# Attention in rounds of waves: Z filled in place in two sets of tiles, scaled keys in halves, new orders of steps

## The reference, cut to what matters

```python
def _attn_ref(q, k, v, beta):            # 4 batches x 8 heads, 768 steps, head size 48
    k_n = k / (np.linalg.norm(k, axis=-1, keepdims=True) + 1e-06)
    state = 0
    for t in range(S):
        y[t] = q[t] @ state
        state = state + beta[t] * outer(k_n[t], v[t] - k_n[t] @ state)

x = attention                            # 3072 tokens x 384
h = x @ w_in;  x = (h * tanh(softplus(h))) @ w_out          # dense stage, 2048 wide
P = exp(x @ w_gate), scaled 8 times by rows and columns
out = sum over 8 experts e of P[:, e] * (relu(x @ w1[e]) @ w2[e])
```

## Time and profile before

| | |
|---|---|
| median of 3 runs (lowest to highest) | 2361.82 us (2361.77 to 2361.85) |
| the profiled execution: time, span | 2361.32 us, 2359.5 us |
| mean granted clock of TensorE | 0.998 |
| busy: TensorE, its weight loads | 2341.0 us (99%), 1960.6 us (83%) |
| busy: VectorE, ScalarE, GpSimd | 1281.0, 838.2, 385.9 us |
| attention, up to its last own matmul | about 0 to 386 us |

### The profile page before, as it was taken

One profiled execution on the slowest core, in us unless ns is written; L12 is line 12 of the kernel. 1 busy time (PEld: TensorE's weight loads), 2 busy tenths in 40 slices (PEclk: granted clock), 3 DMA queues, 4 the chain that ended last, 5 costly groups with the idle time before them and its releaser, 6 DMA issues.

```text
span 2359.5 us, 38749 instructions
## 1 busy us (share of the span) xinstructions
PE 2341.0 (99%) x15924; PEld 1960.6 (83%) x15924; DVE 1281.0 (54%) x2496; ACT 838.2 (36%) x1865; POOL 385.9 (16%) x318
## 2 busy tenths in 40 slices
...
GB/s 95 52 58 61 50 48 56 41 0 0 0 0 28 35 1 56 41 14 45 10 54 41 14 48 7 54 41 14 50 5 54 41 14 50 9 50 43 16 35 68
DMA packets 101298, 82.29 MB, mean 35 GB/s; under 512 B 75136, under 2 KB 82048, under 8 KB 99200
## 3 DMA queue, kind: packets, MB, share of 16 engines
...
q10 hardware_dynamic: 144, 0.20, 0.0%
...
## 4 chain that ended last, share of the span: by engine, by line
PE 93%; DVE 5%; issue 1%; ACT 0%; DMA 0%; POOL 0%; SPq 0%; DVEq 0%; ACTq 0%
PE ex_h L160 46%; PE ex_y L160 45%; PE ex_logits L160 2%; DVE at_X L569 1%; DVE at_gram L512 1%; DVE de_w_lo L908 1%; DVE de_en L923 1%; DVE de_hg L936 1%; PE ex_y L629 0%; DVE de_g_lo L916 0%; DVE at_gram L514 0%; DVE de_en L921 0%; DMA at_k_in<-k 0%; DVE at_Z L572 0%; DVE at_gram L559 0%
## 5 line engine op out<-in xcount | busy, mean ns | idle before, releaser
L1372 DVE SCALAR_TENSOR_TENSOR ex_r_lo<-ex_h,ex_r_hi 128x512 fp32r<-128x512 f32 x384 | 264.3, 688 | 928.5 <-ACT ex_r_hi L1249 928.1
L1249 ACT ACTIVATE ex_r_hi<-ex_h 128x512 fp32r<-128x512 f32 x384 | 229.8, 599 | 1283.8 <-PE ex_h L160 1283.8
L160 PE MATMUL ex_h<-x_hi,ex_w_lo 128*128 128x512 f32 x1152 | 448.7, 389 | 0.0
L160 PE MATMUL ex_h<-x_hi,ex_w_hi 128*128 128x512 f32 x1152 | 448.7, 389 | 0.0
L160 PE MATMUL ex_h<-x_lo,ex_w_hi 128*128 128x512 f32 x1152 | 448.5, 389 | 0.0
L160 PE MATMUL ex_y<-ex_r_lo,ex_w_hi 128*128 128x512 f32 x1152 | 448.2, 389 | 0.0
L160 PE MATMUL ex_y<-ex_r_hi,ex_w_lo 128*128 128x512 f32 x1152 | 448.2, 389 | 0.0
L160 PE MATMUL ex_y<-ex_r_hi,ex_w_hi 128*128 128x512 f32 x1152 | 448.1, 389 | 0.0
L1199 POOL TENSOR_TENSOR ex_w_lo<-ex_stage,ex_w_hi 128x512 fp32r<-128x512 f32 x90 | 115.7, 1287 | 1674.6 <-ACT ex_w_hi L1231 1636.5
L160 PEld LDWEIGHTS ex_h<-x_hi,ex_w_hi 128*128 128x128 f32 x1152 | 216.3, 188 | 45.1 <-issue 0.2
L160 PEld LDWEIGHTS ex_h<-x_hi,ex_w_lo 128*128 128x128 f32 x1152 | 216.3, 188 | 44.9
...
## 6 DMA issues: line engine op xcount, KB each, us to landing
...
```

The source lines that it names most:

```text
L160: return nc.tensor.matmul(out, lhsT, rhs, start=start, stop=stop)
L1249: nc.scalar.activation(r[0][:, j, :], h_bank[j][:], ACT.Relu).then_inc(hi_ready, 1)
L1372: nc.vector.scalar_tensor_tensor(out=r[1][:, j, :], in0=h_bank[j][:], scalar=0.0, in1=r[0][:, j, :].bitcast(F32), op0=ALU.max, op1=ALU.sub ...
```

## The change

Z2 and Z become one array of tiles, a set for even and one for odd waves: ZZ writes the 2x2 blocks into Z, and all products read Z. Step Z0 becomes like the other merges: only the second half of each pair of columns is computed and copied. ZZ now waits for the correction of the wave two before (which frees the set) instead of the Z0 of the wave before. GpSimd scales the keys in two halves, each with a semaphore of its own and a wait for two of the four B4 products; F1.u waits for half u only. The addition of 1e-6 goes from VectorE to ScalarE, behind the root. In the first wave VectorE squares 10 heads and GpSimd 6 instead of 8 and 8; ZZ.2 of the first wave goes from VectorE to GpSimd. Two warm-up matmuls less. `beta_t` lies at another address. The lists of all engines in head, round and last are new. In the round, among others: GpSimd has a rest step (RT.3) between the halves of the keys; the grams of groups 2 and 3 are taken at the beginning of VectorE's next round; on SP loadv comes ahead of loadk. In the last part h1 stands ahead of the last residues (res) instead of behind the last W, and xhi of wave 11 behind g.1 on ScalarE. The numbers of steps of each kind are as before, but for single eZ and eres that change between VectorE and ScalarE (VectorE has 45 eZ instead of 39, of which 5 are Z0, and 20 eres instead of 21).

```diff
 ATTENTION_ROUND = {
     "PE": (
-        "res.1@-1 X5.3@-1 Z5.2@-1 res.0@-1 T5.3@-1 corr.1@-1 res.2@-1 Z5.3@-1 corr.0@-1 F2.3:13 corr.2@-1 H.1 "
-        "res.3@-1 H.0 B2.1@-1:0 H.2 X0.1 X0.0 B2.0@-1:1 T0.0 corr.3@-1 T0.1 B1.1:0 X0.2 Z0.0 Z0.1 B2.3@-1:1 H.3 "
-        "T0.2 X1.0 X1.1 Q.0@-1:3 T1.0 X0.3 T1.1 Z0.2 B2.2@-1:0 Z1.1 Z1.0 T0.3 X1.2 W.0@-1 X2.0 X2.1 T1.2 Z0.3 "
-        "W.1@-1 X1.3 T2.1 Z1.2 T2.0 B4.0@-1:0 B4.3@-1:1 Z2.1 T1.3 Z2.0 B4.1@-1:3 B4.2@-1:2 X3.1 Z1.3 X2.2 X3.0 "
-        "B1.2:0 T3.1 X2.3 T2.2 T3.0 T2.3 Z3.1 Z2.2 F1.1@+1:1 Z3.0 Z2.3 X3.2 X4.1 F1.0@+1:2 X3.3 T3.2 X4.0 T4.1 "
-        "F2.2@+1:01 T3.3 Z3.2 F2.1@+1:32 X4.2 Z4.1 Z3.3 T4.0 F2.0@+1:01 Z4.0 X4.3 T4.2 X5.1 B1.0:3 X5.0 T4.3 "
-        "Z4.2 T5.1 Q.1:2 T5.0 X5.2 Z5.1 Z4.3 B1.3:0 T5.2 Z5.0 "),
+        "Z4.2@-1 Z4.3@-1 corr.0@-1 res.1@-1 X5.2@-1 B1.0@-1:0 X5.3@-1 H.0 T5.2@-1 corr.1@-1 Q.0@-1:2 X0.0 "
+        "Z5.2@-1 H.1 T5.3@-1 B2.1@-1:3 T0.0 X0.1 Z5.3@-1 res.2@-1 Z0.0 res.3@-1 T0.1 X1.0 corr.2@-1 B2.0@-1:0 "
+        "corr.3@-1 T1.0 H.2 Z0.1 B2.2@-1:1 X1.1 H.3 Z1.0 X0.2 B2.3@-1:3 X2.0 T1.1 T0.2 X0.3 W.0@-1 T0.3 Z1.1 "
+        "Q.1@-1:1 Z0.3 T2.0 X2.1 Z0.2 W.1@-1 X1.3 T2.1 Z2.0 X1.2 B4.1@-1:0 B4.0@-1:2 T1.3 X3.0 Z2.1 T1.2 "
+        "B4.2@-1:1 B4.3@-1:3 Z1.3 T3.0 Z1.2 X3.1 F1.0@+1:2 X2.3 X2.2 Z3.0 B1.2:1 T2.3 T3.1 T2.2 X4.0 F2.0@+1:20 "
+        "Z2.2 T4.0 Z2.3 Z3.1 F1.1@+1:1 X3.2 Z4.0 X4.1 X3.3 T3.2 X5.0 F2.1@+1:30 T4.1 T3.3 Z3.2 B1.3:2 T5.0 Z4.1 "
+        "X4.2 B1.1:1 Z3.3 Z5.0 X5.1 F2.2@+1:02 X4.3 T5.1 T4.2 res.0 T4.3 Z5.1 F2.3@+1:31 "),
     "ACT": (
-        "eZ4.0@-1 eT4.2@-1 u4.3@-1 eT4.3@-1 eZ4.2@-1 eT5.1@-1 u5.0@-1 u5.2@-1 eT5.0@-1 eZ5.1@-1 eZ4.3@-1 "
-        "eT5.2@-1 eres.1@-1 u5.3@-1 eT5.3@-1 eZ5.3@-1 u0.0 eH.1 eH.0 eres.3@-1 u0.1 u0.2 eH.2 eT0.0 eT0.1 eZ0.0 "
-        "eZ0.1 eH.3 u1.0 eT0.2 u0.3 u1.1 eT1.0 eT1.1 eZ0.2 eZ1.0 eZ1.1 u1.2 eT0.3 u2.1 xhi.0@-1 u2.0 eZ0.3 eT1.2 "
-        "u1.3 xhi.1@-1 eT2.1 eT2.0 eZ1.2 sqrt@+2 eZ2.1 eT1.3 eZ2.0 u2.2 u3.0 eZ1.3 u3.1 u2.3 eT3.1 eT2.2 eT3.0 "
-        "eT2.3 eZ2.2 eZ3.1 eZ3.0 eZ2.3 eF1.1@+1 u3.2 u4.1 eT3.2 u3.3 eF1.0@+1 u4.0 eT4.1 eZ3.2 eT3.3 eZ3.3 eT4.0 "
-        "eZ4.1 u4.2 u5.1 "),
+        "eres.1@-1 u0.0 eH.0 eT5.2@-1 u5.3@-1 eH.1 eT5.3@-1 u0.1 eT0.0 eZ5.3@-1 eZ0.0 u1.0 eres.3@-1 eT0.1 eT1.0 "
+        "eZ0.1 eH.2 u1.1 eZ1.0 eH.3 u0.2 eT1.1 u0.3 eT0.3 eZ1.1 eT0.2 xhi.0@-1 u2.0 eZ0.3 eZ0.2 eT2.0 u2.1 "
+        "xhi.1@-1 eZ2.0 eT2.1 u1.3 u3.0 u1.2 eT1.3 eT1.2 eZ2.1 eZ1.3 eZ1.2 eT3.0 eF1.0@+1 eZ3.0 u2.2 u3.1 u4.0 "
+        "u2.3 eT2.2 eT3.1 eT2.3 eZ2.2 eT4.0 eZ3.1 eZ2.3 eZ4.0 u5.0 u3.2 eT3.2 eF1.1@+1 u3.3 u4.1 eT4.1 eZ3.2 "
+        "eT3.3 eT5.0 eZ4.1 eZ3.3 u4.2 u4.3 u5.1 eT5.1 sqrt@+2 eT4.2 eZ5.1 eT4.3 eZ4.2 u5.2 eZ4.3 "),
     "DVE": (
-        "gram.7 eX0.0 eX0.1 U.1@-1 U.0@-1 ecorr.3@-1 eX0.2 R.1 U.3@-1 eX1.0 eX1.1 eX0.3 U.2@-1 eX1.2 eX2.0 eX2.1 "
-        "xlo.0@-1 red@+2 eX1.3 xlo.1@-1 st.0@-1 st.3@-1 eX3.1 eX2.2 eX3.0 eX2.3 st.1@-1 R.2 st.2@-1 eX3.2 eX4.1 "
-        "eX3.3 eX4.0 inv@+2 gram.5@+1 gram.4@+1 eX4.2 gram.2@+1 gram.3@+1 eX4.3 eX5.1 eX5.0 R.0 gram.0@+1 eX5.2 "
-        "gram.1@+1 eZ5.0 eX5.3 eZ5.2 eres.0 R.3 eres.2 ecorr.1 ecorr.0 ecorr.2 gram.6@+1 "),
+        "eX4.3@-1 gram.4 eres.0@-1 gram.5 ecorr.0@-1 eX5.2@-1 gram.6 ecorr.1@-1 eX5.3@-1 eX0.0 eZ5.2@-1 R.0@-1 "
+        "gram.7 eX0.1 eres.2@-1 U.1@-1 eX1.0 ecorr.2@-1 U.0@-1 ecorr.3@-1 eX1.1 eX0.2 inv@+1 U.3@-1 eX0.3 U.2@-1 "
+        "eX2.0 xlo.0@-1 eX2.1 eX1.3 eX1.2 xlo.1@-1 st.0@-1 eX3.0 st.1@-1 st.2@-1 eX3.1 eX2.3 eX2.2 red@+2 eX4.0 "
+        "R.2 st.3@-1 gram.1@+1 eX3.2 eX4.1 eX3.3 gram.0@+1 eX5.0 gram.3@+1 R.3 gram.2@+1 eX5.1 eX4.2 eZ5.0 R.1 "),
     "POOL": (
-        "ZZ.3@-2 RT.1@-2 RT.0@-2 kn@-1 RT.3@-2 RT.2@-2 NT.2@-1 NT.1@-1 ZZ.1@-1 NT.0@-1 sq@+1 ZZ.0@-1 ZZ.2@-1 "
-        "NT.3@-1 "),
+        "RT.1@-2 ZZ.2@-2 NT.3@-2 ZZ.3@-2 sq RT.0@-2 RT.2@-2 knh.0@-1 RT.3@-2 knh.1@-1 NT.0@-1 ZZ.0@-1 NT.1@-1 "
+        "ZZ.1@-1 NT.2@-1 "),
     "SP": (
-        "q loadk@+2 loadv "),
+        "q loadv loadk@+2 "),
 }
...
@@ -162,7 +161,7 @@
 FIRST_ROUND = 2
-WARM_UP = 12
+WARM_UP = 10
 BEGUN = 2
 DENSE_STEPS = {"table", "split", "g", "h0", "h1"}
...
@@ -215,8 +214,7 @@
     RT = tiles("RT", range(87, 91), [P, 4, P], F16)
-    Z2 = tiles("Z2_", range(91, 95), [P, 4, P], F16)
-    Z = tiles("Z", range(121, 125), [P, 4, P], F16)
+    Z = [tiles("Z0_", range(91, 95), [P, 4, P], F16), tiles("Z1_", range(121, 125), [P, 4, P], F16)]
     X = tiles("X", range(125, 129), [P, 4, P], F16)
     state = tile("state", 129, [P, B * H // 2, 2 * D])
...
@@ -234,6 +233,7 @@
     HALF = [slice(0, UH // 2), slice(UH // 2, UH)]
+    SPLIT = [slice(10, UH), slice(0, 10)]

     def placed(engine):
...
@@ -318,7 +318,7 @@

-        return tile[:, j, :] if step == ("Z", 0) else pair_half(step[1], step[0] == "Z", tile)[:, j]
+        return pair_half(step[1], step[0] == "Z", tile)[:, j]

     def pair_half(i, second, tile):
...
@@ -326,8 +326,6 @@

-        if step == ("Z", 0):
-            return bank4(bank)
         return bank[:, 0:4 * (P // 2)].rearrange("p (f b c) -> p f b c", f=4, c=MERGES[step[1]])

     def by_parity(ap):
...
@@ -374,7 +372,8 @@
             if kind == "loadk" and n >= W:
-                sp.wait_ge(scaled, 2 * (n - W + 1))
+                for u in range(2):
+                    sp.wait_ge(scaled[u], n - W + 1)
                 load_k(sp, n)
                 for i in (2 * (n - W), 2 * (n - W) + 1):
                     if i < runs:
...
@@ -392,17 +391,14 @@
                 pool.wait_ge(loaded_k[w], 16 * (c + 1))
-                nc.gpsimd.tensor_tensor(square[:, HALF[g]], k_in[w][:, HALF[g]], k_in[w][:, HALF[g]], ALU.mult).then_inc(squared, 1)
-            if kind == "kn":
+                nc.gpsimd.tensor_tensor(square[:, SPLIT[g]], k_in[w][:, SPLIT[g]], k_in[w][:, SPLIT[g]], ALU.mult).then_inc(squared, 1)
+            if kind == "knh":
                 pool.wait_ge(rnorm, n + 1)
                 if n >= W:
-                    for x in range(G):
+                    for x in (2 * g, 2 * g + 1):
                         filled(pool, "B4", x, n - W)
-                nc.gpsimd.tensor_tensor(kn[w][:, :, 0:D], k_in[w][:], by_norm(n), ALU.mult).then_inc(scaled, 2)
-            if kind == "knh":
-                pool.wait_ge(rnorm, n + 1)
                 nc.gpsimd.tensor_tensor(kn[w][:, HALF[g], 0:D], k_in[w][:, HALF[g]], by_norm(n)[:, HALF[g]],
-                                        ALU.mult).then_inc(scaled, 1)
+                                        ALU.mult).then_inc(scaled[g], 1)
             if kind == "NT":
                 if n == 0:
                     pool.wait_ge(masks_in, 16)
...
@@ -412,9 +408,9 @@
                 pool.wait_ge(NT_ready[g], n + 1)
-                if n > 0:
-                    pool.wait_ge(M_filled[g], m_count(n - 1, ("Z", 0)))
-                nc.gpsimd.tensor_tensor(Z2[g][:], NT[w][g][:], four(z2mask), ALU.mult).then_inc(Z2_ready[g], 1)
+                if n >= W:
+                    pool.wait_ge(M_drained[g], m_count(n - W, "corr"))
+                nc.gpsimd.tensor_tensor(Z[w][g][:], NT[w][g][:], four(z2mask), ALU.mult).then_inc(Z2_ready[g], 1)
             if kind == "RT":
                 pool.wait_ge(NT_ready[g], n + 1)
                 if rests:
...
@@ -433,6 +429,8 @@
                 nc.scalar.activation(norm[w][:, 1, :], norm[w][:, 0, :], ACT.Sqrt).then_inc(rooted, 1)
+                act.wait_ge(rooted, n + 1)
+                nc.scalar.activation(norm[w][:, 2, :], norm[w][:, 1, :], ACT.Copy, bias=1e-6).then_inc(biased, 1)
             elif kind == "eF1":
                 filled(act, "F1", g, n)
                 i = o_bank("F1", g, n)
...
@@ -463,7 +461,7 @@
                 else:
-                    to = (T if at[0] == "T" else Z)[g]
+                    to = T[g] if at[0] == "T" else Z[w][g]
                     nc.scalar.copy(changed(at, to), merged(at, M_bank[g])).then_inc(M_drained[g], 1)

         for kind, g, n in steps("ACT"):
...
@@ -484,7 +482,7 @@
                 dve.wait_ge(loaded_k[w], 16 * (c + 1))
-                nc.vector.tensor_tensor(square[:, HALF[g]], k_in[w][:, HALF[g]], k_in[w][:, HALF[g]], ALU.mult).then_inc(squared, 1)
+                nc.vector.tensor_tensor(square[:, SPLIT[g]], k_in[w][:, SPLIT[g]], k_in[w][:, SPLIT[g]], ALU.mult).then_inc(squared, 1)
             elif kind == "red":
                 dve.wait_ge(squared, 2 * (n + 1))
                 nc.vector.tensor_reduce(norm[w][:, 0, :], square[:], AX.X, ALU.add).then_inc(summed, 1)
...
@@ -520,9 +516,7 @@
                 dve.wait_ge(NT_ready[g], n + 1)
-                if n > 0:
-                    dve.wait_ge(M_filled[g], m_count(n - 1, ("Z", 0)))
-                nc.vector.tensor_tensor(Z2[g][:], NT[w][g][:], four(z2mask), ALU.mult).then_inc(Z2_ready[g], 1)
+                nc.vector.tensor_tensor(Z[w][g][:], NT[w][g][:], four(z2mask), ALU.mult).then_inc(Z2_ready[g], 1)
             elif kind == "R":
                 if not first_chunk(n):
```

(30 more changed lines are left out.)

3 lines of the change are left out of this document (2 added, 1 removed), and 125 rows, old and new, of tables (ATTENTION_HEAD, ATTENTION_LAST).

## The result

The changed kernel took 2348.68 us (median of 4 runs, 2348.37 to 2349.03) where the kernel before took 2361.8 (4 runs, 2360.91 to 2361.85): ratio 0.9945, interval 0.993 to 0.996, 13.1 us less. The profiled executions, 2349.03 against 2361.32 us, differ by 12.3, their spans by 12.4. The time forecast was 2352.6: the sign and the range hold, but the gain is 3.9 us larger than the sum, in the region that rival C had.

A forecast was written before the change was run, and what follows sets the result against it. It took TensorE, paid by the column, plus 1.2 us of short waits a round to bound the attention; -5.2 - 2.0 - 1.0 - 1.0 = -9.2 us gave 2352.6 us, range 2345 to 2362.

The forecast's parts named there:

- rival C: Attention rounds: the new orders fit much better, half of the waiting goes, -6 instead of -2 us: 2348.6; chance 0.17.
- Columns, -5.2: Step Z0 on TensorE: 192 matmuls over 12 waves go from 56 to 29 ns each, -5.2 us.
- Waiting in the rounds, -2.0: Attention rounds: new orders, with VectorE and ScalarE lighter, cut TensorE's waiting 0.2 us a round, about ten rounds: -2.0 us.
- Keys in halves, 0, and +0.9 on GpSimd: Scaling of keys: two halves add 0.9 us a round to GpSimd's work; no difference counted in the time.
- 1e-6, small: Addition moved to ScalarE: VectorE loses 812 ns a round, ScalarE gains 0.3 us; pays only through shorter waits.
- Start, -1.0: First wave: fewer warm-up products, F1.0 about 0.8 us earlier, grams can begin 1 us earlier: -1.0 us.
- End, -1.0: Last merges: moving h1 removes the 0.9 us wait for VectorE's split of the weights, perhaps some others: -1.0 us.
- A: Attention rounds: waits take the place of the saved columns, only start and end gain: 2359.8 us; chance 0.17.
- B: Attention rounds: GpSimd's list sets the round, two halves add 8.3 us, so slower: 2368 us; chance 0.08.
- D: Start: TensorE's slow clock lasts longer, a second stretch costing at most 4.1 us: 2356.7 us; chance 0.08.
- E: TensorE: weight loads set the pace, so halving Z0's columns gives nothing, -4.0 us in all: 2357.8; chance 0.05.

The follow-up runs named there:

- the extra half: The changed kernel with GpSimd writing the second half of the scaled keys twice in each wave but the first: 2349.06 us, period 29.57.

## Why the forecast was right in sign and too small

*What bounds it.* TensorE with short waits, as read: the round fell by what its columns and waits fell, and 0.8 us more on GpSimd changed nothing.

*Columns, -5.2.* I counted one pace for all places. Undone in the changed kernel TensorE's part is 2.9 us; the term was too large, because Z0.0, ahead of res.3, saves nothing. The copy, which I gave no term of its own because ScalarE is not full, is 3.5: in the rounds it ends a distance of 0.57 us that X1.0 waits out. The sum of the two, 6.4, lands near 5.2 by luck.

*Waiting in the rounds, -2.0.* The step that was most mis-sized. It is 0.6 us a round, not 0.2 (30.18 to 29.55 by the new lists). I wrote that the orders "can't be worked out from durations alone" and sized the term by the lighter engines, which the runs show to be worth 0 in the old orders and 0.6 us (1e-6) in the new. The shortest distance could have been found blind: X2.3 to T2.3, 0.24 us in the old list, is the place of the largest wait of my own reading, 152.24 us in the earlier trace rows, and the new list has 0.74 us there. It is 0.45 of the 0.6 us; closed again, it costs 0.53. The sum over all distances would have said 0.2, no better than what I took. Rival C, which I gave 0.17, said half of the waiting, -6 us, and ten rounds of 0.6 are that. That its time, 2348.6, fits to 0.1 us is partly luck: start and end gave 2.4 us more than its 2.0 (below), and TensorE's columns 2.3 less than its 5.2.

*Keys in halves, 0, and +0.9 on GpSimd.* Free on GpSimd, but mis-priced: two halves are 2 x 0.83 against 1.48, so +0.18. The only half in the trace of before ran beside VectorE's half. And "no difference" holds in the old orders alone.

*1e-6, small.* Right: 0.6 us by the medians, with the period unchanged. ScalarE's two instructions take 0.22 us each.

*Start, -1.0.* F1.0 began at 8.57, not 8.1, the grams at 11.26, but up to wave 2 the gain is 3.6 us; columns and waits of two waves as forecast (2 x 0.63) leave 2.3. Of these about 1.3 are the warm-up and the split of squares; the rest I put down to the head's order, which no run moved alone.

*End, -1.0.* 392.96 - 350.49 = 42.5 us became 381.25 - 340.16 = 41.1, and 0.7 came behind it: 2.1 together. The 0.9 us wait went as forecast; the waits filled by h1 and the second wait were missed.

*Rivals.* A held in part under the old orders, where 0.30 of the 0.43 us arrived. Under the new ones TensorE's columns gave 0.31, and what is missing to 0.43 is Z0.0's pace and no wait. B is excluded by the extra half. D did not decide: the changed kernel's slow stretch is the shorter one (last section). E had the weight loads set the pace, so that TensorE's columns are worth nothing; they are worth 0.31 us a round, and the starts in the rows above are 0.23 us apart for four matmuls of 128 columns, 57 ns each. The Trainium skill, "TensorE: Matmul & The Clock Gate", section "Back-to-back issue gap", gives about 81 ns for 128 columns in such a stream, and this trace does not agree.
